# First block of a chunked linear-attention kernel: scores in three quarters, one mask a tile, outputs by early, then by late keys

## Chip, cores and metric

One core of one Trainium2 chip. The metric is the device time of one execution in microseconds; of several runs the median is taken. A lower time is better.

## What is computed

The reference is a gated linear attention over 4 batches x 8 heads, 768 tokens, head width 48, and behind it two pairs of dense layers over all 3072 tokens:

```python
for t in range(S):
    state = alpha[:, :, t, :, None] * state + einsum('bhd,bhe->bhde', k[:, :, t], v[:, :, t])
    y[:, :, t] = einsum('bhd,bhde->bhe', q[:, :, t], state)
x = y.transpose(0, 2, 1, 3).reshape(B * S, H * D)         # 3072 x 384
h = x @ w_in;  g = h * clip(h + 3, 0, 6) / 6;  x = g @ w_out      # 384 -> 2048 -> 384
h = x @ w_in2; g = max(h, 0) ** 2;             out = g @ w_out2
```

## The kernel before

**Attention by tiles.** The recurrence is computed in chunks of tokens. `k` and `q` are scaled with running products of the decays, so that inside a chunk `y = (mask of q k^T) v` and between chunks a 48 x 48 state is carried on. There are 18 tiles. Tiles 0 to 3 (`t < BATCH`) are the first block: one tile a batch, with the first 128 tokens of all 8 heads. Tiles 4 to 17 are scored in pieces of 64 tokens, between the steps of the first dense layer. The heads lie in pairs: the even one on rows 0 to 47, the odd one on rows 64 to 111 (`half_rows`). In `k`, `v` and the decays the 128 tokens stand in reversed order, in `q` in natural order. So keys 0 to 63 of a tile are its late keys and 64 to 127 its early ones.

**One tile of the first block.**
- VectorE: `make_decays` (L692 to L713), two scans along the tokens with a reciprocal between them; `scale_keys` for tiles 0 and 3 (L719) and `scale_queries` (L726). GpSimd scales the keys of tiles 1 and 2 (L512).
- TensorE: `score` (L895), 16 matmuls in fp32: per pair of heads, half of the keys (64 of 128 output partitions) and head of the pair one matmul of 48 rows x 64 keys with 128 queries. Even and odd heads go to two PSUM banks. `turn_keys` (L965): four transposes of the keys into a third bank.
- VectorE: `mask` (L744), two multiplications of 128 x 512, one a bank, with the 128 x 128 triangle `causal`, from PSUM to SBUF.
- ScalarE: `copy_keys` (L559) out of PSUM, `check_from_end` and `check_to_token` (L547, L553), which square all decays and add them up for a check of their range, each with a read of its accumulator.
- TensorE: `attend_first` (L973), for each of three groups of output rows four matmuls of all 128 keys x 64 rows with 128 queries; tiles 0 to 2 put all three groups in the bank of their even scores, tile 3 uses three banks. `add_up_first` (L1000): eight matmuls for the tile's state.
- ScalarE: `x_high` or, for tile 3, `last_x_high` (L565) rounds the output to fp32r; `first_state` (L585) copies the state, twice 48 x 192. VectorE: `x_low` and `last_x_low` (L771) take the rest.

**The dense layers.** 96 steps a layer (6 blocks of 512 tokens x 16 groups of 128 hidden columns). A step has `hidden(g)` (L1025, nine fp32r matmuls of 512 columns into `h_ps[g % 2]`) and `project(g - 2)` (L1055, nine more). Between them ScalarE makes `gate(g)` (L592) from PSUM, VectorE the product `activate(g)` (L783), ScalarE its high part `high(g)` (L601), GpSimd its low part `low(g)` (L520). `hidden(g)` waits for `activate(g - 2)`. The weights come in eight groups by DMA; each is split by ScalarE (`split_w`, L619) into a high part and by GpSimd (groups 0 and 1) or VectorE into a low part. `hidden(0)` to `hidden(3)` need group 0, `project(0)` group 1.

**What sets the order.** Each engine runs a list written out by hand and waits only on semaphores: TensorE at L1087 to L1125, VectorE at L832 to L850, ScalarE at L631 to L650, GpSimd at L530 to L535, and SP's queue of transfers at L448 to L480. TensorE's list for the first block is

```python
warm_up(0); score(0); turn_keys(0); warm_up(1); attend_first(0); add_up_first(0)
score(1); turn_keys(1); warm_up(2); attend_first(1); add_up_first(1)
score(2); turn_keys(2); wait_ge(masked, 2); warm_up(3); add_up_first(2)
score(3); turn_keys(3); attend_first(2); attend_first(3); add_up_first(3); hidden(0) ...
```

`warm_up(i)` (L891) issues `WARM_UP[i]` matmuls of 128 x 128 x 128 whose results nobody reads. SP loads tile 6 and later ones into slots of earlier tiles; it waits for both checks and the outputs of the tile that had the slot (`load_tile`, L394).

## Time and profile before

| what | value |
|---|---|
| time, median of 3 runs | 858.87 us (858.85 to 859.05) |
| the profiled execution | 859.79 us, span 858.0 us |
| granted TensorE clock | 1.0 of full speed in all 40 slices |
| TensorE (matmuls) busy | 849.1 us, 99% of the span |
| VectorE busy | 331.7 us, 39% |
| ScalarE busy | 327.7 us, 38% |
| GpSimd busy | 312.0 us, 36% |
| first block, 7.56 to 26.65 us | TensorE 16.89 busy, VectorE 17.28, ScalarE 10.87, GpSimd 8.04 |

The span runs from the first to the last instruction of the profiled execution; the execution's own time has the start and the end around it. "Busy" is the time in which an engine has an instruction in work. A timeline row gives the start, the length from the first start to the last end, the engine, the line of the kernel, the operation, output <- inputs, how many instructions the row stands for, and in brackets the idle time before it with what ended it. The ends of matmuls are modelled, and matmuls overlap: the next start can lie ahead of the end of the one before. An fp32 matmul of the program is two instructions.

### The profile page before, as it was taken

The page shows a single profiled execution, that of the slowest core. Times are in us where ns is not written, and L with a number is a line of the kernel's source. Part 1 is how long each engine was busy: PE and PEld are TensorE (multiplying, and loading weights), DVE is VectorE, ACT ScalarE, POOL GpSimd, SP SyncE. Part 2 cuts the span into 40 slices and gives each one's busy share as a digit, 9 for nine tenths or more (in the row PEclk, how much of TensorE's full clock was granted, in tenths as well). Part 3 has the DMA queues.
Part 4 walks back from the last instruction along what each step waited for, and adds up shares of the span by engine and source line. Part 5 has one row for each costly group of instructions (what it writes and reads, how often), then busy time and mean ns, then how long its engine had stood idle before and what let it go on. Part 6 is the DMA issues. An engine that isn't in the chain of part 4 may idle for free.

```text
span 858.0 us, 15319 instructions
## 1 busy us (share of the span) xinstructions
PE 849.1 (99%) x6312; PEld 703.3 (82%) x6312; DVE 331.7 (39%) x468; ACT 327.7 (38%) x586; POOL 312.0 (36%) x246
## 2 busy tenths in 40 slices
PE   7999999999999999999999999999999999999998
PEld 7888888888888888888888888888888888888886
DVE  8887545564455555421333311212211211211111
ACT  4664433343433334333445433333333333323332
POOL 2655443343443443433333333333333333333332
PEclk9999999999999999999999999999999999999999
DMA  9743233332223332200323001000000000100101
GB/s 347 299 109 94 42 91 90 90 77 74 70 78 103 80 86 75 61 16 5 111 74 111 0 1 38 1 0 25 14 1 7 30 1 0 37 1 1 37 0 39
DMA packets 67496, 51.84 MB, mean 60 GB/s; under 512 B 50785, under 2 KB 57185, under 8 KB 67425
## 3 DMA queue, kind: packets, MB, share of 16 engines
...
## 4 chain that ended last, share of the span: by engine, by line
PE 97%; DMA 1%; SPq 0%; ACT 0%; issue 0%; ACTq 0%
PE h_ps L1051 46%; PE o_ps L1064 46%; PE att_all L944 1%; DMA w_in_raw<-w_in 1%; PE att_all L928 1%; PE att_all L995 1%; PE att_all L1019 1%; SPq L400 0%; PE h_ps L981 0%; ACT k_tok L562 0%; PE att_all L906 0%; SPq L406 0%; PE att_all L981 0%; SPq L402 0%; ACT squares L550 0%
## 5 line engine op out<-in xcount | busy, mean ns | idle before, releaser
L522 POOL TENSOR_TENSOR g_parts<-h_act,g_parts 128x512 fp32r<-128x512 f32 x192 | 256.5, 1336 | 523.9 <-ACT g_parts L604 523.8
L1064 PE MATMUL o_ps<-g_parts,w_out_hi 128*128 128x512 f32 x1152 | 327.1, 389 | 0.0
L1051 PE MATMUL h_ps<-x_parts,w_in_hi 128*128 128x512 f32 x1152 | 295.3, 392 | 0.0
L1064 PEld LDWEIGHTS o_ps<-g_parts,w_out_hi 128*128 128x128 f32 x1152 | 216.2, 188 | 45.0
L1051 PEld LDWEIGHTS h_ps<-x_parts,w_in_hi 128*128 128x128 f32 x1152 | 214.4, 188 | 45.3
L604 ACT ACTIVATE g_parts<-h_act 128x512 fp32r<-128x512 f32 x192 | 121.4, 632 | 272.9 <-PE o_ps L1064 241.0
L790 DVE SCALAR_TENSOR_TENSOR h_act<-h_ps,h_gate 128x512 f32<-128x512 f32 x96 | 66.3, 691 | 290.5 <-ACT h_gate L599 290.5
L1064 PE MATMUL o_ps<-g_parts,w_out_lo 128*128 128x512 f32 x576 | 165.6, 389 | 0.0
L1051 PE MATMUL h_ps<-x_parts,w_in_lo 128*128 128x512 f32 x576 | 161.9, 389 | 0.0
L1051 PEld LDWEIGHTS h_ps<-x_parts,w_in_lo 128*128 128x128 f32 x576 | 108.1, 188 | 22.6
L1064 PEld LDWEIGHTS o_ps<-g_parts,w_out_lo 128*128 128x128 f32 x576 | 108.1, 188 | 22.4
L787 DVE SCALAR_TENSOR_TENSOR h_act<-h_gate,h_ps 128x512 f32<-128x512 f32 x96 | 65.3, 680 | 141.0 <-ACT h_gate L596 141.0
L599 ACT ACTIVATE h_gate<-h_ps 128x512 f32<-128x512 f32 x96 | 57.4, 598 | 110.8 <-PE h_ps L1051 110.8
L596 ACT ACTIVATE h_gate<-h_ps 128x512 f32<-128x512 f32 x96 | 57.2, 596 | 109.2 <-PE h_ps L1051 109.1
L708 DVE TENSOR_TENSOR_SCAN inputs<-inputs,seeds 112x520 f32<-112x520 f32 x18 | 37.0, 2056 | 0.6
L768 DVE TENSOR_TENSOR tails<-att_all,tails 112x128 fp32r<-112x128 f32 x20 | 5.8, 292 | 57.7 <-ACT x_parts L583 57.7
L700 DVE TENSOR_TENSOR_SCAN inputs<-inputs,seeds 112x520 f32<-112x520 f32 x18 | 22.4, 1242 | 1.9
L512 POOL TENSOR_TENSOR inputs<-inputs 112x512 f32<-112x512 f32 x17 | 20.6, 1213 | 0.0
L517 POOL TENSOR_TENSOR inputs<-inputs 112x512 f32<-112x512 f32 x17 | 20.4, 1197 | 0.0
L810 DVE TENSOR_TENSOR x_parts<-x_mid,x_parts 128x1536 fp32r<-128x1536 f32 x6 | 10.6, 1759 | 18.3 <-ACT x_parts L625 18.3
L741 DVE STREAM_TRANSPOSE x_mid<-inputs 128x512 f32<-128x512 f32 x16 | 17.5, 1092 | 0.0
L944 PEld LDWEIGHTS att_all<-inputs,state 48*48 48x48 f32 x576 | 11.3, 120 | 6.6 <-issue 6.3
...
## 6 DMA issues: line engine op xcount, KB each, us to landing
...
```

Source lines behind the costliest of these rows:

```text
L512: nc.gpsimd.tensor_tensor(by_chunk(t, keys(t)), by_chunk(t, keys(t)), from_end(t)[:, :, 0:chunk(t)], ALU.mult).then_inc(k_scaled, 1)
L517: nc.gpsimd.tensor_tensor(by_chunk(t, queries(t)), by_chunk(t, queries(t)), to_token(t)[:, :, 0:chunk(t)], ALU.mult).then_inc(q_scaled, 1)
L522: nc.gpsimd.tensor_tensor(g_parts[:, g % 2, 1, :], h_act[:, g % 2, :], g_parts[:, g % 2, 0, :].bitcast(F32), ALU.subtract).then_inc(g_lo, 1)
L596: nc.scalar.activation(h_gate[:, g % 2, :], h_ps[g % 2][:, :], ACT.Relu, bias=0.5, scale=1.0 / 6.0).then_inc(gate_made, 1)
L599: nc.scalar.activation(h_gate[:, g % 2, :], h_ps[g % 2][:, :], ACT.Relu).then_inc(gate_made, 1)
L604: nc.scalar.activation(g_parts[:, g % 2, 0, :], h_act[:, g % 2, :], ACT.Copy).then_inc(g_hi, 1)
L700: nc.vector.tensor_tensor_scan(scanned(t, ATT_W), scanned(t, KQ_W), other_seeds(t), 0.0, ALU.mult, ALU.max).then_inc(from_end_made, 1)
L708: nc.vector.tensor_tensor_scan(loaded[:, ::-1], loaded[:, ::-1], other_seeds(t), 0.0, ALU.mult, ALU.max).then_inc(to_token_made, 1)
L787: nc.vector.scalar_tensor_tensor(h_act[:, g % 2, :], h_gate[:, g % 2, :], 1.0, h_ps[g % 2][:, :], ALU.min, ALU.mult).then_inc(act_made, 1)
L790: nc.vector.scalar_tensor_tensor(h_act[:, g % 2, :], h_ps[g % 2][:, :], 0.0, h_gate[:, g % 2, :], ALU.max, ALU.mult).then_inc(act_made, 1)
L1051: last = nc.tensor.matmul(h_ps[g % 2][:, :], w[:, m, cols], x_parts[:, n % 2, part, m, :], start=m == 0 and i == 0, stop=m == KT - 1 and i ...
L1064: return nc.tensor.matmul(o_ps[m][:, :], w[:, f, m * P:(m + 1) * P], g_parts[:, g % 2, part, :], start=f == 0 and w is w_out_hi and part = ...
```

## The change

- **Scores in three quarters.** `score` leaves out the quarter of late keys by early queries, which the mask makes zero. The other three are written as three kinds, one after the other: late keys by late queries, early keys by early queries, both to columns 0 to 255 of the tile's two banks (on partitions 0 to 63 and 64 to 127), then early keys by late queries to columns 256 to 511. Within a kind it goes over the four pairs and their two heads: 24 matmuls of 64 columns, with one `scored` at the end of either bank.
- **One mask.** VectorE multiplies both diagonal quarters of both banks in one operation of 128 x 512 with the 64 x 64 triangles `causal_part`. ScalarE's new `copy_cross` copies the third quarter (64 x 512) to SBUF, after the mask. `causal` and its two GpSimd operations are gone.
- **Outputs in two passes.** `attend_first` first does the 12 matmuls of the early keys (64 rows, all 128 queries), then waits for them (`early_attended`) and adds the 12 of the late keys (64 rows, 64 late queries) to the same sums. Tile 3, with its banks of its own, waits group by group. It also waits for `cross_copied`.
- **Order.** TensorE: `warm_up(3)` and its wait for `masked` go; `turn_keys(2)`, `turn_keys(3)`, `score(3)`, `add_up_first(2)` follow each other. ScalarE: the four `copy_cross`; `split_w(0)` behind `copy_cross(1)`, `split_w(1)` behind the last high part, `check_to_token(1)` behind `first_state(3)`, and the checks of tiles 2 and 3 one step of the first layer later.
- **Banks.** All of PSUM is one tensor, and the first block's scores, keys, sums and outputs are given to other banks (`FIRST_BANKS`, `FIRST_Y_BANK`, `LAST_Y_BANKS`). Outputs: tile 0's in the bank of its odd scores, tile 2's in the one of its even scores.

```diff
--- before.py
+++ after.py
...
+BANK = 512
+H_BANK, O_BANK, ATT_BANK = 0, 2, 5
...
+FIRST_BANKS = ((ATT_BANK, ATT_BANK + 1, ATT_BANK + 2), (O_BANK + 1, O_BANK + 2, O_BANK), (H_BANK, H_BANK + 1, ATT_BANK + 2),
+               (O_BANK + 2, ATT_BANK, O_BANK))
+FIRST_Y_BANK = (ATT_BANK + 1, O_BANK + 1, H_BANK)
+LAST_Y_BANKS = (H_BANK + 1, O_BANK + 2, ATT_BANK)
 SCORES_W = PAIRS * PART
...
-WARM_UP = (14, 8, 3, 2)
+WARM_UP = (14, 8, 3)
...
-            return pairs(banks(t)[2][half_rows(half), 0:PAIRS * HD])
...
+        def bank(n):
+            return banks[:, n * BANK:(n + 1) * BANK]
+        def first_bank(t, i):
+            return bank(FIRST_BANKS[t][i])
+        def first_scores(t, rows, first):
+            even, odd = FIRST_BANKS[t][0:2]
+            part = banks[rows, even * BANK + first:even * BANK + first + SCORES_W]
+            return bass.AP(part.tensor, part.offset, [part.ap[0], [(odd - even) * BANK, 2], [PART, PAIRS], [1, PART]])
         def first_y(t, m):
-            bank = (att_ps[1], o_ps[1], att_ps[0])[m] if t == BATCH - 1 else banks(t)[0]
-            return bank[:, m * TILE:(m + 1) * TILE]
+            return bank(LAST_Y_BANKS[m] if t == BATCH - 1 else FIRST_Y_BANK[t])[:, m * TILE:(m + 1) * TILE]
...
         def by_part(ap):
             return ap.rearrange("p m (a q) -> p m a q", a=2)
+        LATE, EARLY = slice(0, PART), slice(PART, TILE)
...
+        cross_copied = sem("cross_copied")
+        early_attended = sem("early_attended")
...
             nc.gpsimd.memset(ident[:], 0.0).then_inc(init_pool, 1)
-            nc.gpsimd.memset(causal[:], 1.0).then_inc(init_pool, 1)
-            pool.wait_ge(init_pool, 2)
+            pool.wait_ge(init_pool, 1)
             nc.gpsimd.affine_select(out=ident[:], in_=ident[:], compare_op=ALU.not_equal, fill=1.0, base=0,
                                     pattern=[[-1, P]], channel_multiplier=1).then_inc(init_pool, 1)
-            nc.gpsimd.affine_select(out=causal[:], in_=causal[:], compare_op=ALU.is_ge, fill=0.0, base=1 - TILE,
-                                    pattern=[[1, TILE]], channel_multiplier=1).then_inc(init_pool, 1)
-            pool.wait_ge(init_pool, 4)
+            pool.wait_ge(init_pool, 2)
             nc.gpsimd.memset(state[:, :, :, :], 0.0).then_inc(state_cleared, 1)
             nc.gpsimd.memset(causal_part[:], 1.0).then_inc(part_ready, 1)
             pool.wait_ge(part_ready, 1)
...
                 past(act, u_made, t)
-                nc.scalar.activation(k_tok[:, :, :], banks(t)[2][:, 0:PAIRS * ROWS].rearrange("p (a b) -> p a b", a=PAIRS),
+                nc.scalar.activation(k_tok[:, :, :], first_bank(t, 2)[:, 0:PAIRS * ROWS].rearrange("p (a b) -> p a b", a=PAIRS),
                                      ACT.Copy).then_inc(k_back_copied, 1)
+            def copy_cross(t):
+                act.wait_ge(masked, 2 * (t + 1))
+                nc.scalar.activation(masked_of(t)[EARLY, :, :, PART:TILE], first_scores(t, EARLY, SCORES_W), ACT.Copy).then_inc(cross_copied, 1)
...
             copy_keys(0)
             check_from_end(0)
             check_to_token(0)
+            copy_cross(0)
             x_high(0)
             first_state(0)
-            split_w(0)
             copy_keys(1)
             check_from_end(1)
-            check_to_token(1)
+            copy_cross(1)
+            split_w(0)
             x_high(1)
             first_state(1)
             copy_keys(2)
-            split_w(1)
+            copy_cross(2)
+            copy_cross(3)
             copy_keys(3)
             x_high(2)
             for m in range(KT):
                 last_x_high(m)
+            split_w(1)
             first_state(2)
             first_state(3)
-            check_from_end(2)
+            check_to_token(1)
             for g in range(2 * STEPS + LAG):
                 n, f = divmod(g, FT)
                 if g < 2 * STEPS:
                     gate(g)
                     if g == 0:
+                        check_from_end(2)
+                    if g == 1:
                         check_to_token(2)
-                    if g == 1:
+                    if g == 2:
                         check_from_end(3)
-                    if g == 2:
+                    if g == 3:
                         check_to_token(3)
...
             def mask(t):
-                for half in range(2):
-                    dve.wait_ge(scored, 2 * t + half + 1)
-                    past(dve, y_made, t - 1)
-                    nc.vector.tensor_tensor(masked_of(t)[:, half, :, :], pairs(banks(t)[half][:, :]),
-                                            causal[:, :].unsqueeze(1).broadcast_to([P, PAIRS, TILE]), ALU.mult).then_inc(masked, 1)
+                dve.wait_ge(part_ready, 3)
+                dve.wait_ge(scored, 2 * (t + 1))
+                past(dve, y_made, t - 1)
+                nc.vector.tensor_tensor(masked_of(t)[:, :, :, 0:PART], first_scores(t, slice(0, P), 0),
+                                        causal_part[:, :].unsqueeze(1).unsqueeze(1).broadcast_to([P, 2, PAIRS, PART]),
+                                        ALU.mult).then_inc(masked, 2)
             def mask_later(t):
-                if t == BATCH:
-                    dve.wait_ge(part_ready, 3)
                 dve.wait_ge(scored, pieces_of(t))
                 dve.wait_ge(y_made, t)
...
-            dve.wait_ge(init_pool, 4)
...
             def warm_up(i):
-                for _ in range(WARM_UP[i]):
-                    nc.tensor.matmul((att_ps[1] if i == 3 else h_ps[0])[:, 0:P], ident[:, :], ident[:, :], start=True, stop=True)
+                for n in range(WARM_UP[i]):
+                    place = att_ps[n // 2][:, 256 + n % 2 * P:256 + (n % 2 + 1) * P] if i == 0 and n < 4 else h_ps[0][:, 0:P]
+                    nc.tensor.matmul(place, ident[:, :], ident[:, :], start=True, stop=True)
...
             def score(t):
-                bank_even, bank_odd, _ = banks(t)
                 pe.wait_ge(k_scaled, t + 1)
                 pe.wait_ge(q_scaled, t + 1)
                 if t == BATCH - 1:
                     pe.wait_ge(masked, 2 * (t - 1))
-                for j in range(PAIRS):
-                    for part in range(2):
-                        cols = slice(HALF * part, HALF * (part + 1))
-                        for half, bank in enumerate((bank_even, bank_odd)):
+                    pe.wait_ge(cross_copied, t - 1)
+                for kind, (keys_of, queries_of, first) in enumerate(((LATE, slice(PART, TILE), 0), (EARLY, slice(0, PART), 0),
+                                                                     (EARLY, slice(PART, TILE), SCORES_W))):
+                    for j in range(PAIRS):
+                        for half in range(2):
                             rows = half_rows(half)
-                            last = nc.tensor.matmul(bank[cols, j * TILE:(j + 1) * TILE], keys(t)[rows, j, cols],
-                                                    queries(t)[rows, j, :], start=True, stop=True)
-                            if j == PAIRS - 1 and part == 1:
+                            last = nc.tensor.matmul(first_bank(t, half)[keys_of, first + j * PART:first + (j + 1) * PART],
+                                                    keys(t)[rows, j, keys_of], queries(t)[rows, j, queries_of], start=True, stop=True)
+                            if kind == 2 and j == PAIRS - 1:
                                 last.then_inc(scored, 1)
...
             def turn_keys(t):
-                bank_k = banks(t)[2]
+                pe.wait_ge(k_scaled, t + 1)
+                bank_k = first_bank(t, 2)
                 if t >= 2:
                     pe.wait_ge(state_made, 2 * (t - 1))
                 for j in range(PAIRS):
...
             def attend_first(t):
                 wait_values(pe, t)
                 pe.wait_ge(masked, 2 * (t + 1))
+                pe.wait_ge(cross_copied, t + 1)
                 for m in range(KT):
-                    if t == BATCH - 1 and m == KT - 1:
-                        pe.wait_ge(x_lo, 1)
                     for kind, j in enumerate((m, TAIL)):
                         for half in range(2):
                             last = nc.tensor.matmul(first_y(t, m)[HALF * half:HALF * (half + 1), :],
-                                                    first_values(t)[:, kind, m, half, :], masked_of(t)[:, side_of(j, half), j, :],
-                                                    start=kind == 0, stop=kind == 1)
+                                                    first_values(t)[EARLY, kind, m, half, :], masked_of(t)[EARLY, side_of(j, half), j, :],
+                                                    start=kind == 0 and (m == 0 or t == BATCH - 1), stop=True, skip_group_check=True)
+                    last.then_inc(early_attended, 1)
+                for m in range(KT):
+                    pe.wait_ge(early_attended, KT * t + (m + 1 if t == BATCH - 1 else KT))
+                    for kind, j in enumerate((m, TAIL)):
+                        for half in range(2):
+                            last = nc.tensor.matmul(first_y(t, m)[HALF * half:HALF * (half + 1), PART:TILE],
+                                                    first_values(t)[LATE, kind, m, half, :], masked_of(t)[LATE, side_of(j, half), j, 0:PART],
+                                                    start=False, stop=True, skip_group_check=True)
                     if t == BATCH - 1 and m < KT - 1:
                         last.then_inc(last_y_made, 1)
                 last.then_inc(y_made, 1)
...
-            pe.wait_ge(init_pool, 4)
+            pe.wait_ge(init_pool, 2)
             pe.wait_ge(init_vec, 1)
             warm_up(0)
             score(0)
...
             add_up_first(1)
             score(2)
             turn_keys(2)
-            pe.wait_ge(masked, 2)
-            warm_up(3)
+            turn_keys(3)
+            score(3)
             add_up_first(2)
-            score(3)
-            turn_keys(3)
             attend_first(2)
             attend_first(3)
             add_up_first(3)
...
```

## Rows read from the trace of the kernel before

**Rows 1.** Page, parts span and 1: busy time and share of each engine.

```profile
span 858.0 us, 15319 instructions
...
PE 849.1 (99%) x6312; PEld 703.3 (82%) x6312; DVE 331.7 (39%) x468; ACT 327.7 (38%) x586; POOL 312.0 (36%) x246
```

**Rows 2.** TensorE's waits from 22 us on: total us, times, longest.

```profile
PE att_all L928 <- PE att_all L995: 0.2, 1, 0.2
```

**Rows 3.** Timeline of TensorE, 0 to 46 us: start, length, instructions, idle before.

```profile
7.56 1.10 PE L906 MATMUL att_all<-x_mid 48*64 48x128 f32 x32 [0.66 <-DVE x_mid L726]
8.59 0.60 PE L970 MATMUL att_all<-ident,x_mid 112*128 112x112 f32 x4
...
11.58 1.53 PE L981 MATMUL att_all<-masked_t,first_v 128*64 128x128 f32 x24 [0.58 <-DVE masked_t L748]
12.91 0.56 PE L1009 MATMUL att_all<-first_v,k_tok 128*48 128x48 f32 x16
13.40 1.10 PE L906 MATMUL o_ps<-x_mid 48*64 48x128 f32 x32
...
16.39 1.53 PE L981 MATMUL o_ps<-h_gate,first_v 128*64 128x128 f32 x24 [0.67 <-DVE h_gate L748]
...
20.50 0.62 PE L893 MATMUL att_all<-ident 128*128 128x128 f32 x4
...
26.20 0.53 PE L1009 MATMUL o_ps<-first_v,k_tok 128*48 128x48 f32 x16
26.65 1.65 PE L1051 MATMUL h_ps<-x_parts,w_in_hi 128*128 128x512 f32 x6
...
30.86 1.52 PE L1051 MATMUL h_ps<-x_parts,w_in_hi 128*128 128x512 f32 x6
...
44.31 0.63 PE L995 MATMUL att_all<-masked_t,inputs 64*48 64x64 f32 x32
45.13 0.70 PE L928 MATMUL att_all<-inputs 48*64 48x64 f32 x32 [0.19 <-PE att_all L995]
45.62 0.43 PE L944 MATMUL att_all<-inputs,state 48*48 48x64 f32 x16
```

**Rows 4.** The same timeline inside the scores of tile 3.

```profile
22.12 0.27 PE L906 MATMUL att_all<-x_mid 48*64 48x128 f32 x1
...
22.14 0.27 PE L906 MATMUL o_ps<-x_mid 48*64 48x128 f32 x1
22.23 0.27 PE L906 MATMUL att_all<-x_mid 48*64 48x128 f32 x1
```

**Rows 5.** Timeline of VectorE: masks, and products of the first layer.

```profile
10.17 1.26 DVE L748 TENSOR_TENSOR masked_t<-att_all,causal 128x512 f32<-128x512 f32 x2
...
14.98 1.26 DVE L748 TENSOR_TENSOR h_gate<-o_ps,causal 128x512 f32<-128x512 f32 x2
...
29.66 0.69 DVE L787 SCALAR_TENSOR_TENSOR h_act<-h_gate,h_ps 128x512 f32<-128x512 f32 x1 [0.61 <-ACT h_gate L596]
...
33.89 0.67 DVE L787 SCALAR_TENSOR_TENSOR h_act<-h_gate,h_ps 128x512 f32<-128x512 f32 x1
...
41.88 0.68 DVE L756 TENSOR_TENSOR masked_t<-att_all,causal_part 128x512 f32<-128x512 f32 x1
```

**Rows 6.** Timeline of ScalarE: key copy, check, gate, weight split.

```profile
9.30 0.54 ACT L562 ACTIVATE k_tok<-att_all 128x448 f32<-128x448 f32 x1 [6.99 <-PE att_all L970]
...
11.09 0.19 ACT L556 ACTIVATION_READ_ACCUMULATOR squares<-x_mid 112x1 f32 x1
...
29.02 0.60 ACT L596 ACTIVATE h_gate<-h_ps 128x512 f32<-128x512 f32 x1 [0.33 <-PE h_ps L1051]
...
35.14 1.47 ACT L621 ACTIVATE w_in_hi<-w_in_raw 128x1536 fp32r<-128x1536 f32 x1
```

**Rows 7.** Timeline of GpSimd: the low part of a weight group.

```profile
24.41 3.48 POOL L527 TENSOR_TENSOR w_out_lo<-w_out_raw,w_out_hi 128x1536 fp32r<-128x1536 f32 x1
```

**Rows 8.** Line L708 by form, VectorE's second scan: lengths min/median/max in ns.

```profile
L708 DVE TENSOR_TENSOR_SCAN inputs<-inputs,seeds x18: 1241/2239/2242, 30.5 to 357.4; 112x520 f32<-112x520 f32 x18
```

22 lines of the change are left out of this document (9 added, 13 removed).

## Prediction

> **What bounds the kernel now.** The page comes first. TensorE is busy for 99% of the span [rows 1]. Its waits from 22 us to the end hold one entry, 0.2 us [rows 2]. So everything from the first product of the first layer, `hidden(0)` at 26.65 us, to the end is TensorE's own work, which the change leaves alone. An edit of the first block can move the time in two ways: it shifts the start of `hidden(0)`, or it makes one of the first steps behind it wait.
>
> Next, TensorE's timeline up to 26.65 us [rows 3]. It is nearly full: the idle bits in front of the first scores and the outputs of tiles 0 and 1 are 0.66, 0.58 and 0.67 us, and warm-ups, such as the one of 0.62 at 20.50 which the change drops, fill time that nothing else wanted. Their end-to-start order shows the pace: scores, key turn, warm-up, wait for the mask, outputs, sums, next scores. VectorE runs in a closed line beside it [rows 5]: the first mask starts at 10.17 although its scores ended at 8.66, the second at 14.98 although its scores ended at 14.50. Up to there VectorE sets the pace. From the scores of tile 3 on TensorE has no gap at all [rows 2]. So both engines are near the limit in this stretch, and the question is which one the change loads.
>
> **Unit prices of TensorE.** The matmuls of the scores start four at a time, every 0.11 us [rows 4]: the four quarters of the array (two key-row halves by two output halves) run side by side, and each quarter takes one instruction of 128 columns in 0.107 us. An fp32 matmul is two instructions (16 matmuls are x32). 64 columns take half: 32 instructions of `score_later`, eight a quarter, go from 45.13 to the next start at 45.62 [rows 3], 0.43 us at 0.053 each plus a little. The outputs use two quarters' worth at a time (all 128 rows, two column halves): 24 instructions, 12 a half, 12 x 0.107 = 1.28 us, and 11.58 to 12.91 shows 1.33.
>
> **Scores.** Before: 32 instructions over four quarters, 8 x 0.107 = 0.86; start to next start 1.03 [rows 3]. After: 24 matmuls, 48 instructions of 64 columns. But the kind is the outer loop, and within a kind all go to one output half, so only two quarters work: 24 x 0.053 = 1.28, less one pair that overlaps where late keys give way to early ones: 1.23. So each score costs 0.37 to 0.38 more, though it computes a quarter less. Start to next is 1.41, start to ready 1.48 instead of 1.10.
>
> **Outputs, the largest term.** Before 1.33. After, the early keys' pass has 64 rows but still 128 columns and two column halves: 1.28, its last result at +1.53 (its row's length). Then TensorE waits for its own semaphore `early_attended`. The one such wait in the trace, `attended` before `score_later`, left it idle 0.19 us after the drained end (44.31 + 0.63 to 45.13) [rows 2, 3]. Late keys' pass: 24 instructions of 64 columns on two quarters, 12 x 0.053 = 0.64. Sum: 1.53 + 0.19 + 0.64 = 2.36. Behind it the sums use another division of the array than these 64-row pieces. Such changes cost: from scores to key turn it is 1.03 for 0.86 of work, some 0.15 [rows 3]. The Trainium skill says the same ("TensorEngine Tiling (Array Packing)", Key Properties: a change of tiling mode drains the engine); without it the sum would be 0.15 x 4 = 0.6 smaller. So start to next is 2.51, +1.18 for each of tiles 0, 1 and 2, all queued in front of the tile's sums and the next tile's scores. Tile 3 has a bank for each output and waits only for the same `m`, so no drain: 1.28 + 0.64 + 0.15 = 2.07 against 1.31, +0.75.
>
> **VectorE.** Two multiplications a tile, 1.26 us, become one of as many elements as `mask_later` has, 0.68 at 41.88 [rows 5]: 0.6 less a tile, four times. That pays only where VectorE sets the pace.
>
> **ScalarE.** `copy_cross`: 512 elements out of PSUM as in `gate`, 0.60 [rows 6], and it waits for the whole mask. So the path from scores to outputs is not shorter: 0.68 + 0.04 + 0.60 + 0.06 against 1.26 + 0.15. It is also queued behind the key copy and one or both checks. Before, from a key copy to the end of both checks it took 9.30 to 11.28, 1.89 to the next start [rows 6].
>
> **The line through the first block**, each time from the ones before:
> - scores(0) start at 7.56 as now (VectorE's queries). Next start 8.97, keys turned 9.57.
> - ScalarE: key copy 9.62, checks, `copy_cross(0)` 11.51 to 12.11. Outputs(0) 12.17 (11.58 now). The mask was ready at 10.85, so the ScalarE queue decides here.
> - Sums(0) 14.68, scores(1) 15.17 (13.40 now), ready 16.65. VectorE could have masked at 14.40 and stands idle for 2.3 us: TensorE is the pace now. Mask(1) 16.70 to 17.38.
> - Keys(1) turned 17.18; ScalarE: copy 17.22 and one check, 1.06 for both (0.44 for the copy, its length of 0.54 less the overlap, and less than half of what is left of the 1.89, since the wait between two checks falls away), `copy_cross(1)` 18.28 to 18.88. Outputs(1) 18.94 (16.39 now).
> - Sums(1) 21.45, scores(2) 21.94 (sums take 0.49 as 12.91 to 13.40), key turns(2, 3) 23.35, scores(3) 24.30 (two turns of 0.60 less overlap and a change of division),  sums(2) 25.71, outputs(2) 26.20. Beside this VectorE, from mask(1) at 16.70, is ready for mask(2) after the 4.81 that lie between the masks now [rows 5], less 0.6 for the halved mask and plus 0.6 for its own keys of tile 3: 21.5, before scores(2) are ready at 23.42. Mask(3) starts at 25.8, and its copy ends at 27.2, before outputs(3) wants it.
> - Outputs(3) 28.56, sums(3) 30.63, `hidden(0)` 31.08 with the 0.45 now seen from 26.20 to 26.65.
>
> Shift of `hidden(0)`: 31.08 - 26.65 = **+4.4 us**. The warm-up of 0.62 that is dropped and the lost idle bits are in this already. A check by adding up: 4 x 0.38 + 3 x 1.18 + 0.75 = 5.8, plus 0.6 and 0.8 that ScalarE's queue adds in front of outputs(0) and (1), less some 2.8 of warm-up and idle time that are eaten.
>
> **The first steps behind it.** ScalarE now has `split_w(1)` (1.47 long, 1.38 to the next, as the split at 35.14 [rows 6]) between the last high part and `first_state(2)`. Before, `gate(0)` started at 29.02, 2.37 after `hidden(0)`, of which 0.33 was idle: the queue was ready at +2.04. In the line above the last high part falls 0.1 earlier against `hidden(0)` than now, so the queue is ready at 2.04 + 1.38 - 0.1 = +3.3. `gate(0)` ends at +3.9, VectorE's product at +4.6, TensorE may go at +4.75, and `hidden(2)` was due at +4.21 (30.86 [rows 3]): 0.5 lost. VectorE then has the decays of tile 4 before the next product (29.66 to 33.89, 4.23 apart [rows 5]), so `hidden(3)` loses another 0.1. GpSimd's low part of that weight group (3.48 [rows 7]) starts at +1.5 and ends at +5.0, before `project(0)`, which comes after a third hidden product at +6.7. The two checks moved a step later, and the checks that SP's loads of tiles 6 and 7 wait for, cost nothing: tile 6's load needs tile 0's checks and outputs alone, and tile 7's stands in SP's queue behind `store_turned(4)`, which needs work of the first layer's fourth step, when tile 1's late check (34 us) is long done. GpSimd's shorter start gives TensorE its first warm-up 0.4 us earlier, which ends in more waiting for VectorE at 7.56: nothing.
>
> **Sum.** 4.4 + 0.6 = +5.0 us. The profiled execution took 859.79 us for a span of 858.0; the median of the runs is 858.87, 0.92 lower. By the profile: span 863.0, execution 864.8. By the median: 858.87 + 5.0 = **863.9 us**.
>
> **Unknown prices.** The wait for its own pass: nothing, if it drains beside other work, to twice the 0.44 (0.25 of drain, 0.19 idle): -1.3 to +1.3 over three tiles; I take the row, the same kind of wait. Change of division: 0 to 0.19: -0.6 to +0.2. Steps behind `hidden(0)`: 0 to 1.4, since VectorE's second scan may run beside GpSimd, where most of its kind took 2.24 instead of 1.24 [rows 8]. One output half with two row halves never runs alone in this trace: between four quarters' pace (0.64 a score, below now) and none side by side (2.5); I take two, since the four starts of a group include such pairs.
>
> **Rivals.**
> - *The late pass does not wait* (chance 0.14): drain and change of division hidden. Then outputs cost 1.33 + 0.64, `hidden(0)` comes near 29.5 and the time is 862.3. For it: starts overlap the ends before them everywhere. Against it: the one self-wait in the trace did idle.
> - *Not slower* (0.12): the parts that use different rows run side by side, late keys beside early ones, in scores and outputs. This decides once a tile's outputs cost no more than 1.33 and a score 0.82. Then VectorE stays the pace and its 0.6 a tile counts: the same line gives `hidden(0)` at 24.6 for both, 26.95 if only the outputs gain. With 0.6 behind it: 857.4 to 859.8. The Trainium skill gives the principle ("TensorE: Matmul & The Clock Gate", Part 3: matmuls on different row groups run at the same time). Against it: the late pass adds to the same sums and has a wait ahead of it, and the starts go in program order with the kind outermost. Only tile 3 has its own banks, and there I let the passes overlap.
> - *ScalarE and VectorE late in the first layer* (0.08): the scan beside GpSimd adds 0.8 to the product that `hidden(3)` wants, and the queue of copies adds as much again: 865.7.
>
> My forecast has 0.66. Its own range is 862.9 to 865.0. The range that holds 8 in 10 reaches to the first rival's lower half and to the third's time: 861.0 to 865.7. A measurement of this kernel can tell 0.2%, 1.7 us. Faster by more: 0.04 (the lower end of the second rival). Within: 0.08. Slower: 0.88.
>
> **What would show it.** Right: outputs of tiles 0 to 2 in two groups with about 0.2 us of idle time released by TensorE itself; each score 1.4 to the next start; VectorE idle more than 1.5 us before mask(1), released by TensorE; `hidden(0)` near 31.1; a wait of about half a microsecond of `hidden(2)` for VectorE. Wrong: late matmuls that start beside early ones in tiles 0 to 2, scores in under 1 us, or `hidden(0)` before 27.

## The result and the profile after

The changed kernel took **875.66 us** (median of 6, 867.90 to 876.97), the kernel before 858.94 in the same comparison: a ratio of 1.016, interval 1.013 to 1.019. It is slower, as forecast, but by 16.7 us in the median where 5.0 was forecast, and outside the range of 861.0 to 865.7.

The six times fall into two groups, and the granted TensorE clock goes with them:

```
us      867.90  868.09  874.75  876.57  876.86  876.97
clock   1.000   1.000   0.986   0.982   0.982   0.982
```

Executions of the kernel before, seven of them listed with the first experiments, all had 1.000 (the 24 listed with the later ones had 0.999 or 1.000). The granted clock is the one that TensorE was given, averaged over the execution, as a share of full speed (2.4 GHz). The profiled execution is the one of 867.90 us. Its page [rows 1]:

```profile
span 866.2 us, 15633 instructions
...
PE 854.8 (99%) x6468; PEld 708.0 (82%) x6468; DVE 331.0 (38%) x464; ACT 330.3 (38%) x590; POOL 312.2 (36%) x244
```

TensorE's waits from 10 us on, total, times, longest, without the one entry of 0.2 us that [rows 2] had and that is still there:

```profile
PE banks L1010 <- ACT h_gate L585: 1.3, 1, 1.3
PE banks L1010 <- ACT masked_t L585: 1.0, 1, 1.0
PE banks L1010 <- issue: 1.0, 1, 1.0
PE banks L934 <- issue: 0.8, 1, 0.8
PE banks L1088 <- DVE h_act L813: 0.8, 2, 0.4
```

Two entries name "issue": TensorE waited for nothing that the profile shows. The forecast had neither. They are called the unnamed gaps from here on.

TensorE's timeline, the counterpart of [rows 3] (L934 scores, L999 key turn, L1010 early pass, L1018 late pass, L1046 sums, L1088 `hidden`):

```profile
7.56 1.44 PE L934 MATMUL banks<-x_mid 48*64 48x64 f32 x48 [0.61 <-DVE x_mid L753]
8.94 0.60 PE L999 MATMUL banks<-ident,x_mid 112*128 112x112 f32 x4
...
12.38 1.53 PE L1010 MATMUL banks<-masked_t,first_v 64*64 64x128 f32 x24 [1.04 <-ACT masked_t L585]
13.96 0.92 PE L1018 MATMUL banks<-masked_t,first_v 64*64 64x64 f32 x24
14.81 0.56 PE L1046 MATMUL banks<-first_v,k_tok 128*48 128x48 f32 x16
15.30 1.44 PE L934 MATMUL banks<-x_mid 48*64 48x64 f32 x48
...
19.23 1.78 PE L1010 MATMUL banks<-h_gate,first_v 64*64 64x128 f32 x24 [1.27 <-ACT h_gate L585]
...
22.42 1.44 PE L934 MATMUL banks<-x_mid 48*64 48x64 f32 x48
...
24.70 0.44 PE L934 MATMUL banks<-x_mid 48*64 48x64 f32 x7
25.91 1.21 PE L934 MATMUL banks<-x_mid 48*64 48x64 f32 x41 [0.76 <-issue]
...
32.16 0.32 PE L1010 MATMUL banks<-h_gate,first_v 64*64 64x128 f32 x1 [0.97 <-issue]
...
33.52 1.66 PE L1088 MATMUL banks<-x_parts,w_in_hi 128*128 128x512 f32 x6
...
38.21 1.67 PE L1088 MATMUL banks<-x_parts,w_in_hi 128*128 128x512 f32 x6 [0.32 <-DVE h_act L813]
...
43.06 1.66 PE L1088 MATMUL banks<-x_parts,w_in_hi 128*128 128x512 f32 x6 [0.43 <-DVE h_act L813]
```

`hidden(0)` starts at 33.52 instead of 26.65: +6.9, where +4.4 was forecast. `hidden(2)` and `hidden(3)` are idle for 0.32 and 0.43 us before they start. Up to the scores of tile 2 the forecast line holds within half a microsecond: 8.94 (8.97), 12.38 (12.17), 15.30 (15.17), 19.23 (18.94), 22.42 (21.94). It breaks inside the scores of tile 3: seven instructions from 24.70, then nothing until 25.91. A second gap lies in front of 32.16, inside the outputs of tile 3. The early pass of tile 1 at 19.23 is also 0.25 longer than that of tile 0 (1.78 for 1.53).

VectorE's mask of tile 1 [rows 5]; the idle time before it was forecast at 2.3 us and is 1.85, released by TensorE:

```profile
16.92 0.69 DVE L775 TENSOR_TENSOR h_gate<-banks,causal_part 128x512 f32<-128x512 f32 x1 [1.85 <-PE banks L934]
```

ScalarE [rows 6]: `copy_cross(0)`, `split_w(1)`, `gate(0)`:

```profile
11.64 0.59 ACT L585 ACTIVATE masked_t<-banks 64x512 f32<-64x512 f32 x1
...
33.32 1.48 ACT L643 ACTIVATE w_out_hi<-w_out_raw 128x1536 fp32r<-128x1536 f32 x1
...
36.83 0.60 ACT L618 ACTIVATE h_gate<-banks 128x512 f32<-128x512 f32 x1
```

`gate(0)` starts 3.31 us after `hidden(0)`, as forecast (+3.3). So the profiled execution has the forecast mechanism, plus two unnamed gaps, and four of six executions have something else besides.

### The profile page after: what moved, and what is told of

It reads as the page before. It is cut to its first block, busy times and chain, and to the rows that moved or that the text cites. A ratio compares the mean times of both kernels' runs of the same rounds, so it can differ in the third digit from the quotient of the medians.

```text
span 866.2 us, 15633 instructions
## 1 busy us (share of the span) xinstructions
PE 854.8 (99%) x6468; PEld 708.0 (82%) x6468; DVE 331.0 (38%) x464; ACT 330.3 (38%) x590; POOL 312.2 (36%) x244
## 4 chain that ended last, share of the span: by engine, by line
PE 97%; DVE 1%; ACT 1%; issue 1%; DMA 0%; ACTq 0%
PE banks L1088 45%; PE banks L1101 45%; PE banks L972 1%; PE banks L956 1%; PE banks L1032 1%; PE banks L1056 1%; PE banks L1010 1%; PE banks L934 1%; PE banks L1018 0%; DMA x_mid<-att_in 0%; PE banks L999 0%; DVE inputs L735 0%; DVE inputs L746 0%; PE banks L1046 0%; ACT squares L573 0%
## 5 line engine op out<-in xcount | busy, mean ns | idle before, releaser
L1101 PE MATMUL banks<-g_parts,w_out_hi 128*128 128x512 f32 x1152 | 327.1, 389 | 0.0
L1088 PE MATMUL banks<-x_parts,w_in_hi 128*128 128x512 f32 x1152 | 295.7, 392 | 0.8 <-DVE h_act L813 0.8
L1101 PEld LDWEIGHTS banks<-g_parts,w_out_hi 128*128 128x128 f32 x1152 | 216.3, 188 | 44.8
L1088 PEld LDWEIGHTS banks<-x_parts,w_in_hi 128*128 128x128 f32 x1152 | 214.4, 188 | 46.7 <-DVE h_act L813 1.6
L816 DVE SCALAR_TENSOR_TENSOR h_act<-banks,h_gate 128x512 f32<-128x512 f32 x96 | 66.3, 691 | 290.5 <-ACT h_gate L621 290.5
L1101 PE MATMUL banks<-g_parts,w_out_lo 128*128 128x512 f32 x576 | 165.7, 389 | 0.0
L1088 PE MATMUL banks<-x_parts,w_in_lo 128*128 128x512 f32 x576 | 162.0, 390 | 0.0
L1088 PEld LDWEIGHTS banks<-x_parts,w_in_lo 128*128 128x128 f32 x576 | 108.2, 188 | 22.7
L1101 PEld LDWEIGHTS banks<-g_parts,w_out_lo 128*128 128x128 f32 x576 | 108.2, 188 | 22.5
L621 ACT ACTIVATE h_gate<-banks 128x512 f32<-128x512 f32 x96 | 57.5, 599 | 110.8 <-PE banks L1088 110.8
L618 ACT ACTIVATE h_gate<-banks 128x512 f32<-128x512 f32 x96 | 57.3, 597 | 107.9 <-PE banks L1088 107.9
L972 PEld LDWEIGHTS banks<-inputs,state 48*48 48x48 f32 x576 | 11.3, 120 | 6.6 <-issue 6.3
```

The source lines that it names most:

```text
L618: nc.scalar.activation(h_gate[:, g % 2, :], h_ps[g % 2][:, :], ACT.Relu, bias=0.5, scale=1.0 / 6.0).then_inc(gate_made, 1)
L621: nc.scalar.activation(h_gate[:, g % 2, :], h_ps[g % 2][:, :], ACT.Relu).then_inc(gate_made, 1)
L816: nc.vector.scalar_tensor_tensor(h_act[:, g % 2, :], h_ps[g % 2][:, :], 0.0, h_gate[:, g % 2, :], ALU.max, ALU.mult).then_inc(act_made, 1)
L1088: last = nc.tensor.matmul(h_ps[g % 2][:, :], w[:, m, cols], x_parts[:, n % 2, part, m, :], start=m == 0 and i == 0, stop=m == KT - 1 and i ...
L1101: return nc.tensor.matmul(o_ps[m][:, :], w[:, f, m * P:(m + 1) * P], g_parts[:, g % 2, part, :], start=f == 0 and w is w_out_hi and part = ...
```

## Experiments

Twelve experiments ran. Those named a_ are the changed kernel again or edits of it, those named b_ edits of the kernel before. Three things were to be settled: the unnamed gaps, the clock, and how the forecast's own terms share the rest.

### a_again: the changed kernel once more, to see a trace at the low clock

> The changed kernel once more, unchanged. Its times so far lie in two groups, 867.9 to 868.1 us at a granted clock of 1.000 and 874.8 to 877.0 at 0.982 to 0.986. Theory: the 8.8 us between the groups is one stretch of TensorE at 1.2 GHz that begins in the first 40 us; expected again both groups, and, if the profiled execution is one of the slow ones, a stretch in its trace in which a product of 512 columns takes about 0.43 us instead of 0.23. Rival: the runs differ in something else (transfers, the end of the kernel) and the mean clock only goes with it; then the low clock is spread or lies late.

Four executions: 876.68, 876.51, 873.15 and 868.54 us at clocks of 0.982, 0.982, 0.988 and 0.995. The profiled one was the first. Its time in stretches (the columns after the busy times are granted clock, DMA share, GB/s):

```profile
12.00:14.00 2.00, 1.31 (x24) 1.31 (x24) 1.82 (x5) 0.55 (x1) 0.00 (x0) 1.00 0.97 382
14.00:16.00 2.00, 1.94 (x38) 1.61 (x36) 1.07 (x1) 0.32 (x1) 0.84 (x1) 0.63 1.05 406
16.00:40.00 24.00, 23.22 (x322) 21.14 (x322) 8.01 (x13) 7.95 (x16) 3.77 (x2) 0.50 0.90 354
...
44.00:46.00 2.00, 2.00 (x8) 1.58 (x7) 0.37 (x1) 1.34 (x4) 2.00 (x1) 0.69 0.01 4
46.00:60.00 14.00, 14.00 (x92) 11.36 (x91) 13.06 (x16) 10.24 (x20) 8.60 (x5) 1.00 0.01 2
```

TensorE's rows at both ends of the stretch:

```profile
12.69 1.53 PE L1010 MATMUL banks<-masked_t,first_v 64*64 64x128 f32 x24 [1.03 <-ACT masked_t L585]
14.28 1.36 PE L1018 MATMUL banks<-masked_t,first_v 64*64 64x64 f32 x24
...
42.43 2.93 PE L1088 MATMUL banks<-x_parts,w_in_hi 128*128 128x512 f32 x6
...
45.89 1.53 PE L1088 MATMUL banks<-x_parts,w_in_hi 128*128 128x512 f32 x6
```

The early pass of tile 0 at 12.69 has its full-clock length (1.53), the late pass at 14.28 takes 1.36 for 0.92. From 14.6 the granted clock is 0.50 (1.2 GHz) until 45.2. All the small matmuls of the first block run at it, 322 of them from 16 to 40 us with TensorE busy for 23.22 of 24 us, and in this execution none brings the clock back. It comes back behind the first six products of 128 rows, 128 columns of weights and 512 columns of data (2.93 for them at 42.43, 1.53 at 45.89). `hidden(0)` starts at 42.43 instead of 33.52, and the span is 8.8 longer. The rival (a difference elsewhere in the kernel) falls: the shift of `hidden(0)` is 8.9 and that of the end 8.8. Two things do differ besides. The first warm-up takes 6.21 us where the other profiled execution has 5.21, and the first scores start 0.32 later. And the unnamed gaps (1.7 us idle) and the two waits of `hidden(2)` and `hidden(3)` (0.75 us) are gone in this execution, so that the slow stretch costs more than 8.8 by itself. That the gaps are gone because TensorE consumes its code more slowly is a likely reason, not tested by itself.

### a_held: no weight transfers beside the first block

```diff
             load_values(4)
+            sp.wait_ge(y_made, BATCH)
             load_w(2)
             load_w(3)
```

> The changed kernel with SP's queue held before load_w(2) until tile 3's outputs are made, so that no weight transfers run beside the first block from about 20 us on. Theory (instruction fetch): the two idle stretches that TensorE's rows put down to nothing (0.8 us inside the scores of tile 3, 1.0 us inside its outputs) are instruction blocks of 16 KB that come late through busy DMA engines; with the engines free both vanish and hidden(0) starts near 31.4 us instead of 33.5. The later steps keep their time unless a weight group comes late, so 866 us in the fast group. Rival (a wait for another engine or for sums that the profile doesn't name): both idle stretches stay as they are, hidden(0) at 33.5.

In the profiled execution (865.39 us, clock 1.0), scores of tile 3 and `hidden(0)`:

```profile
24.68 1.44 PE L935 MATMUL banks<-x_mid 48*64 48x64 f32 x48
...
31.14 1.66 PE L1089 MATMUL banks<-x_parts,w_in_hi 128*128 128x512 f32 x6
```

Both gaps are gone; the 48 instructions of the scores are in one piece, and `hidden(0)` starts at **31.14**. The forecast had 31.08. The span is 2.5 us shorter than the changed kernel's. Instruction blocks have a queue of their own in the trace. One of the changed kernel's, from 23.0 to 23.5 us (packets, MB, share of 16 engines' time):

```profile
q8 instruction: 1, 0.02, 12.9%
```

In quarters of a microsecond, such packets show from 16.0, 23.25 and 29.5 us in the changed kernel, with the DMA engines full (a share of 1.03 from 16 to 32 us); in a_held from 16.0, 20.75, 24.75 and 29.5, with a share of 0.24 from 20 to 25 us. The gaps end at 25.91 and 32.16, 2.7 us behind the packets' start. Between the two gaps lie 127 matmuls with a weight load each, 254 instructions. The Trainium skill describes this ("Runtime: NRT & Kernel Launch", Instruction fetch mechanics: an engine's code is refilled in blocks of 16 KiB, 256 instructions); the trace agrees with the size (0.02 MB a packet) and nearly with the spacing. The same section calls the cost mostly hidden; here `hidden(0)` came 2.4 us later for it. The long early pass of tile 1 (1.78), whose slack lies some 124 matmuls ahead of the first gap, looks like a third and smaller one. It stays in a_held, where the DMA engines are still full up to 20 us. The other three executions still fell to 0.989, 0.988 and 0.982 (871.72 to 876.80 us), so the hold does nothing for the clock.

### a_four: diagonal quarters of the scores interleaved

```diff
-                for kind, (keys_of, queries_of, first) in enumerate(...):
-                    for j in range(PAIRS):
-                        for half in range(2):
+                for j in range(PAIRS):
+                    for keys_of, queries_of in ((LATE, slice(PART, TILE)), (EARLY, slice(0, PART))):
+                        for half in range(2):
+                            piece(j, half, keys_of, queries_of, 0)
+                for j in range(PAIRS):
+                    for half in range(2):
+                        last = piece(j, half, EARLY, slice(PART, TILE), SCORES_W)
```

> The changed kernel with the late and the early diagonal quarter of the scores interleaved pair by pair, so that four quarters of the array work for two thirds of the matmuls. Theory (a kind has only two quarters of the array): a score takes 1.05 us to the next start instead of 1.38, because 16 matmuls of 64 columns on four quarters take 0.43 and the other 8 on two take 0.43; hidden(0) about 0.9 to 1.2 us earlier if no instruction block is later for it, else the gain is lost in longer idle stretches. Rival (the number of instructions sets the pace, 48 at some 29 ns): the score stays at 1.38 to 1.44 us.

Scores of tile 0 and what follows:

```profile
7.62 1.16 PE L931 MATMUL banks<-x_mid 48*64 48x64 f32 x48 [0.67 <-DVE x_mid L753]
8.72 0.60 PE L1004 MATMUL banks<-ident,x_mid 112*128 112x112 f32 x4
```

1.10 to the next start instead of 1.38, with as many instructions. So the forecast's price was right: a kind by itself has only two of the array's quarters, and two instructions side by side take 0.053 us. Of four times 0.28, `hidden(0)` gained 0.83 (32.69), and the gap in the scores of tile 3 grew from 0.76 to 0.96. Times: 867.35, 867.38, 867.60 at 0.998 and 871.95 at 0.988. In the profiled execution the clock fell at 32.9, beside the first products of the dense layer, and was back at 36.3. Three of the four executions lost so little; whether the denser scores are the reason was not tested.

### b_more: more instructions in the warm-ups of the kernel before

```diff
-                for _ in range(WARM_UP[i]):
-                    nc.tensor.matmul(...[:, 0:P], ident[:, :], ident[:, :], ...)
+                pieces = 4 if i else 1
+                for _ in range(WARM_UP[i] * pieces):
+                    nc.tensor.matmul(...[:, 0:P // pieces], ident[:, :], ident[:, 0:P // pieces], ...)
```

> The kernel before with warm_up(1) to (3) in pieces of 32 columns, 52 matmuls in place of 13 of 128 columns: the same columns, 78 trace matmuls (156 instructions) more. Theory (instruction fetch): the block boundary falls into the scores or outputs of tile 3 and TensorE idles there for 0.3 to 1.5 us with nothing named as the cause, so the time is 859.2 to 860.4 us, and some executions may fall to a lower clock. Rival (no fetch limit): no unnamed idle stretch, 858.9 us plus at most 0.5 for the overhead of small matmuls.

869.31 us median, and it tests nothing of instruction fetch. Each of the added matmuls has a load of 128 columns of weights. At full clock 24 of them took 2.78 us (0.116 each), about what one of 128 columns takes (16 in 1.96, 0.122 each). `warm_up(1)`, with 64 for 16, took 9.04 us, and the clock fell in it:

```profile
9.60 9.04 PE L894 MATMUL h_ps<-ident 128*128 128x32 f32 x64
18.57 2.83 PE L982 MATMUL att_all<-masked_t,first_v 128*64 128x128 f32 x24
```

TensorE was slower by more than the added code could make up, and no unnamed gap appeared. The expectation had priced the columns and not the weight loads. The run shows something else, though: the granted clock is at 0.50 from 14.8 to 21.5 us, and TensorE had stood idle nowhere between 8.12 us and that fall. It came back while the outputs and sums of tile 0 ran, on all 128 rows.

### a_fill: longer warm-ups in front of the outputs of tiles 0 and 1

```diff
-WARM_UP = (14, 8, 3)
+WARM_UP = (14, 12, 8)
```

> The changed kernel with warm_up(1) of 12 matmuls instead of 8 and warm_up(2) of 8 instead of 3, which fills 0.85 of the 1.04 us and 1.07 of the 1.27 us that TensorE stands idle before the outputs of tiles 0 and 1. Theory (those idle bits, beside matmuls that use half of the array's rows, let the clock fall to 1.2 GHz): granted clock 1.000 in all executions or nearly all, 867 to 869 us each, no group at 875. The nine matmuls more put the late instruction blocks a little earlier in the code, so the two unnamed idle stretches stay at 0.8 to 1.5 us. Rival (the short and narrow matmuls alone are too little activity, whatever lies between them): most executions still at 0.98 to 0.99 and 872 to 877 us.

**866.02 us**, four executions from 865.83 to 866.32, all at a clock of 1.000; a little under the expected 867, since the late blocks cost less too. Nine matmuls whose results nobody reads take 9.6 us off the median. The early pass of tile 1, with 0.16 us of idle time before it instead of 1.27, and `hidden(0)`:

```profile
19.33 1.53 PE L1010 MATMUL banks<-h_gate,first_v 64*64 64x128 f32 x24 [0.16 <-ACT h_gate L585]
...
31.61 1.64 PE L1088 MATMUL banks<-x_parts,w_in_hi 128*128 128x512 f32 x6
```

Waits, of which only the second unnamed gap is left, and half as long:

```profile
PE banks L1010 <- issue: 0.4, 1, 0.4
```

`hidden(0)` at 31.61 is nearly a_held's, with full DMA engines. A likely reason: the filler runs in time that was idle, so TensorE reaches the end of a code block earlier, and the next one is asked for earlier. The traces bear it out. The instruction packets show from 12.0, 19.25 and 26.75 us instead of 16.0, 23.25 and 29.5. And the gap that is left lies 18 matmul instructions earlier in the code than the second one before, which is just what nine more matmuls of two instructions each move a block's end by. So the gaps go with a place in the code and not with a certain wait. As to the clock, a_fill ran on another chip than the changed kernel in a_again. But on a third chip a_split (below), with these warm-ups and other edits besides, had 0.999 to 1.000 in all four executions, and a_fill_one, without the longer second warm-up, fell to 0.988 in two of four.

### a_fill_one: only the first warm-up longer

```diff
-WARM_UP = (14, 8, 3)
+WARM_UP = (14, 12, 3)
```

> The changed kernel with warm_up(1) alone lengthened, 12 matmuls for 8; the 1.27 us of idle time before the outputs of tile 1 stay. Theory: either idle bit is enough to let the clock fall, so some executions still end up at 0.985 to 0.99 (the fall comes at about 21 us instead of 14.5) and 870 to 875 us. Rival: the first bit, near the start of the full clock, is what counts; then all stay at 1.000 and 866 to 868 us.

865.70 and 865.78 us at 1.000 and 0.999, 872.94 and 873.27 at 0.988. So the clock still falls in some executions with the second idle bit (1.27 us) alone; no slow one of this kernel was profiled, so the place of the fall isn't shown. In the profiled one (865.70) four more matmuls did as much against the unnamed gaps as holding the transfers back: packets from 12.25, 19.25 and 26.75 us, no "issue" among the waits, the early pass of tile 1 in 1.53 and

```profile
31.16 1.67 PE L1088 MATMUL banks<-x_parts,w_in_hi 128*128 128x512 f32 x6
```

with the DMA engines as full as before (shares of 1.00 to 1.07 from 16 to 36 us).

### b_cold and b_two_cold: idle time with and without the narrower matmuls

```diff
-WARM_UP = (14, 8, 3, 2)
+WARM_UP = (14, 0, 3, 2)
```

> The kernel before without warm_up(1), so that TensorE stands idle for some 2.5 us before the outputs of tile 0. Theory (an idle stretch in the first block makes the clock fall, and the first block's own matmuls don't bring it back): the clock falls to 1.2 GHz there and stays there until the products of the dense layer, as in the slow executions of the changed kernel; mean clock about 0.98 to 0.99 and 862 to 868 us. Rival (only the changed kernel's 64-row pieces keep the clock down): the clock is back within the first block, and the time is 859 to 861 us.

The theory as I had put it fell: 858.97 us (10 executions, 858.73 to 860.20), clock 0.998 to 1.000, although TensorE is idle for 2.39 us before the outputs of tile 0. Four of the ten had 0.998 and 859.62 to 860.20 us, the others at most 858.98, so the clock may have fallen for a short stretch in those; none of them was profiled. Idle time alone does not keep it down. The same edit on b_two (below), where nothing but the outputs differs from b_cold:

> The kernel before with outputs in two passes (b_two) and without warm_up(1). b_two alone never left the full clock, and the kernel before without warm_up(1) hardly did. Theory: it takes both, idle time of more than a microsecond and matmuls on half of the rows behind it; then the clock falls in most executions and stays at 1.2 GHz until the dense layer, mean clock 0.98 to 0.99, 866 to 872 us. Rival (the scores on two quarters keep it down, not the outputs): clock 0.998 to 1.000 and 861.5 to 864 us.

870.54 us median (864.83 at 0.996, the other three 870.41 to 870.75 at 0.988):

```profile
12.00:16.00 4.00, 3.94 (x50) 3.42 (x47) 3.02 (x5) 0.00 (x0) 0.72 (x1) 0.50 1.04 403
16.00:30.00 14.00, 13.93 (x168) 12.12 (x170) 7.03 (x11) 6.64 (x14) 3.89 (x2) 0.50 1.03 404
30.00:34.00 4.00, 4.00 (x70) 3.44 (x70) 1.37 (x3) 1.47 (x2) 3.00 (x1) 0.70 1.05 407
```

The clock is down from 12.0, just behind the start of the outputs of tile 0 (11.72), and comes back at 32.4, at the end of the scores of tile 3, which here still use all four quarters. The same scores of tiles 1 and 2 had not brought it back. b_two itself, with its idle bits of 0.59 and 0.27 us, had 1.000 in all six executions. So in these kernels it takes both: the idle time of 2.4 us, and behind it the outputs in two passes on half of the rows. Two things limit this. b_two and b_cold ran on one chip and b_two_cold on another, so that a difference between chips isn't excluded here. And it is no rule: in b_more the clock fell with no idle time and all rows in use. And the two passes differ from the one in more than their rows, they also take 1.1 us longer, so which of it counts isn't separated.

### b_two: the kernel before with outputs in two passes

```diff
-    first_values(t)[:, kind, m, half, :], masked_of(t)[:, side_of(j, half), j, :], ...
+    first_values(t)[PART:TILE, kind, m, half, :], masked_of(t)[PART:TILE, side_of(j, half), j, :], ...
+    last.then_inc(early_attended, 1)
+for m in range(KT):
+    pe.wait_ge(early_attended, ...)
+    ... first_y(t, m)[..., PART:TILE], first_values(t)[0:PART, ...], masked_of(t)[0:PART, ..., PART:TILE]
```

> The kernel before with one part of the change alone: outputs in two passes of 64 keys, the second over the 64 late queries after a wait for the first. Scores, masks and ScalarE's queue as before. Theory: each of tiles 0 to 2 takes 2.45 instead of 1.33 us for its outputs, tile 3 2.0 instead of 1.3; VectorE's line still sets the masks of tiles 0 and 1, so about half of 4.1 us is eaten by the warm-ups' and waits' room: hidden(0) at 29.0 to 30.0 instead of 26.65, 861.4 to 862.6 us at clock 1.000. Rival (the scores and the ScalarE copies cost most of the 4.5 us): hidden(0) before 28 and under 860.5 us. If the clock falls in some executions here too, it is the 64-row outputs that bring it about, not the copies' waits.

862.10 us (862.02 to 862.62), ratio 1.0036 (1.0024 to 1.0049). Outputs of tile 0 in two passes, sums, and `hidden(0)`:

```profile
11.67 1.53 PE L982 MATMUL att_all<-masked_t,first_v 64*64 64x128 f32 x24 [0.59 <-DVE masked_t L749]
...
14.10 0.56 PE L1018 MATMUL att_all<-first_v,k_tok 128*48 128x48 f32 x16
...
29.22 1.65 PE L1060 MATMUL h_ps<-x_parts,w_in_hi 128*128 128x512 f32 x6
```

2.43 to the sums (11.67 to 14.10) where the forecast had 2.51, and `hidden(0)` 2.6 later. This one part costs 3.1 us (862.10 against 859.03); the whole change was forecast at 5.0.

### a_between: sums between the two passes

```diff
                     last.then_inc(early_attended, 1)
+                if between:
+                    add_up_first(t)
                 for m in range(KT):
```

with the hold of a_held and the warm-ups of a_fill.

> The changed kernel with the held weight transfers, the longer warm-ups of a_fill, and the sums of tiles 0 to 2 issued between the early and the late pass of the outputs, so that they stand in for the drain. Theory (the pass of late keys waits 0.19 us beyond the drained end of the early pass, some 0.4 us of TensorE in all, for each of three tiles): outputs and sums of a tile together take 2.45 to 2.5 us instead of 2.92 (12.38 to 15.30), hidden(0) at 30.0 to 30.4 instead of 31.14 us, clock 1.000, 864.0 to 864.8 us. Rival (the self-wait costs nothing beyond the pipeline's end, or two changes of the array's division eat the gain): hidden(0) at 30.9 or later and 865 us.

864.63 us (864.60 to 864.93), clock 1.000. Tile 0, early pass, sums, late pass, next scores:

```profile
12.68 1.53 PE L1011 MATMUL banks<-masked_t,first_v 64*64 64x128 f32 x24
14.13 0.56 PE L1049 MATMUL banks<-first_v,k_tok 128*48 128x48 f32 x16
14.63 0.85 PE L1021 MATMUL banks<-masked_t,first_v 64*64 64x64 f32 x21
...
15.37 1.40 PE L935 MATMUL banks<-x_mid 48*64 48x64 f32 x47
```

12.68 to 15.37 is 2.69 for outputs and sums, where the changed kernel needs 2.92 (12.38 to 15.30). `hidden(0)` comes at 30.38 instead of 31.14. The time around the self-wait (TensorE's wait for its own early pass) is real and can be filled, but the saving is 0.23 in tile 0 and not 0.4. The expectation's 2.45 to 2.5 had left out the two changes of the array's division, which is a likely reason and was not tested; its start for `hidden(0)` was met, in part because tile 1's early pass took 1.53 here and 1.78 in a_held.

### a_split: split_w(1) moved in front of x_high(2)

```diff
             copy_keys(3)
+            split_w(1)
             x_high(2)
             for m in range(KT):
                 last_x_high(m)
-            split_w(1)
```

> a_between with ScalarE's split_w(1) moved from behind the last high part to in front of x_high(2), where ScalarE stood idle. Theory: the two waits of hidden(2) and hidden(3) for VectorE (0.30 and 0.49 us, with the drained pipeline about 1.1 us together) come from the ScalarE queue in front of gate(0) alone; both go, hidden(0) stays at 30.4, and the time falls from 864.6 to 863.5 us. Rival (VectorE itself is late with the decays of tile 4): the second wait stays, 864.1 us or more.

863.70 us (863.43 to 863.80) after 864.63 in a_between. TensorE's waits, apart from the first, are now three, of 0.4, 0.2 and 0.2 us, and none of them is one of `hidden(2)` or `hidden(3)` for VectorE. The place of the split in ScalarE's queue cost 0.9 us, nearly all of it behind `hidden(0)` (30.25 for 30.38).

### a_all: all repairs together

```diff
             check_from_end(0)
+            copy_cross(0)
             check_to_token(0)
-            copy_cross(0)
             ...
-WARM_UP = (14, 8, 3)
+WARM_UP = (14, 10, 5)
```

and the edits of a_held, a_four, a_between and a_split.

> All repairs of the changed kernel together: held weight transfers, sums between the passes, diagonal quarters of the scores interleaved, split_w(1) in front of x_high(2), copy_cross(0) and (1) in front of the last check, warm-ups of 10 and 5. By the line of times: outputs(0) 11.65, scores(1) 14.3, outputs(1) 17.25, scores(2) 19.9, scores(3) 21.9, outputs(3) 25.45, hidden(0) 27.9 us against 26.65 in the kernel before, no wait behind it. Theory: 860.2 us (859.6 to 861.0), clock 1.000, still slower than before, since TensorE's two passes cost 0.64 a tile more than VectorE's relief is worth. Rival (VectorE was what held the first block, and the relief counts once the queues are in order): under 858.5 us.

862.13 us median; four executions lie from 861.38 to 862.79 at 1.000, one at 862.69 (0.999) and one at 867.33 (0.994). Outputs of tiles 0 and 1, and `hidden(0)`:

```profile
11.65 1.53 PE L1016 MATMUL banks<-masked_t,first_v 64*64 64x128 f32 x24
...
17.33 1.53 PE L1016 MATMUL banks<-h_gate,first_v 64*64 64x128 f32 x24 [0.21 <-ACT h_gate L586]
...
28.08 1.66 PE L1096 MATMUL banks<-x_parts,w_in_hi 128*128 128x512 f32 x6
```

The expected line had 11.65, 17.25 and 27.9, but the profiled execution took 861.38 us where 860.2 was expected. So the line is right, and the mapping to the time a microsecond too good: I had taken the start of `hidden(0)` in the profiled execution before, 26.65, for that of the median, and that execution lay 0.9 us above the median. With all queues in order the change is still 2.4 us slower in its best execution and 3.1 in the median. No version that beats the kernel before was found.

## Why the prediction failed

**Where the 16.7 us are.** The profiled execution of 867.90 us lies 9.0 above the median before. Against the profiled execution before, `hidden(0)` is 6.9 later and 1.3 is lost behind it, 8.2 together; that execution was itself 0.9 above its median. Of the 6.9, 4.5 are the forecast line (31.14 in a_held against 26.65), and 2.4 the late instruction blocks. The median lies another 7.8 above 867.90, since most executions have a stretch at 1.2 GHz.

| term | forecast | measured | by |
|---|---|---|---|
| line of scores, outputs and copies up to `hidden(0)` | +4.4 | +4.5 | a_held |
| late instruction blocks | - | +2.4 | a_held |
| first steps of the dense layer | +0.6 | +1.3 | after; 0.9 of it a_split |
| profiled execution before, above its median | - | +0.9 | before |
| clock at 1.2 GHz in most executions | - | +7.8 in the median | a_again, a_fill |

The rows are rounded. The last one is the net of the fall: 8.8 in the span of a_again, in which the gaps and the waits of the first steps are gone. Against a_held's profiled execution, which has no such gaps, a_again is 11.3 longer.

**Step by step.**
- *What bounds the kernel*: right that TensorE and not VectorE is the pace, and that the line of TensorE's work up to `hidden(0)` is what counts. Wrong in what it took as given: TensorE's prices of [rows 3] hold only at the clock of that trace and with the code at hand. This is the step that failed: a fall of the clock and late code were terms put at nothing, without a reason. The runs showed in their place a granted clock of 0.50 from 14.6 to 45.2 us in a_again, 8.8 us of its span, and 2.4 us of late code. Warm-ups were read as filling "time that nothing else wanted"; in this kernel they also keep up the clock. a_fill shows it at a cost of nine matmuls: 866.02 for 875.66 us.
- *Scores*: +0.35 to the next start (1.38 against 1.03), forecast +0.38. Shown by a_four.
- *Outputs*: +1.10 (2.43 against 1.33), forecast +1.18. The self-wait: the late pass starts 1.58 behind the early one (12.38 to 13.96), so it idles by 0.05 and not by 0.19 past the modelled end. Tile 3 overlapped its passes as forecast (1.97 to its sums in a_held, forecast 2.07).
- *ScalarE*: `copy_cross(0)` at 11.64 (11.51), outputs(0) 12.38 (12.17): ScalarE's copy reaches TensorE 0.15 us after its end, not 0.06. The idle bits that it left, 1.04 and 1.27 us, were in the forecast's line (outputs(0) 0.6 later, the warm-up's length unchanged), but priced at nothing beyond themselves.
- *VectorE*: the masks were halved as forecast (0.67 for 1.26), but the query scaling behind mask(0) took 1.47 for 0.87, so the idle time in front of mask(1) is 1.85 and not 2.3. TensorE was the pace there, so it cost nothing.
- *From the line to the time*: the forecast took +5.0 to the median, 858.87, and dropped the 864.8 that it had by the profile. But its line gives times of the trace, and 26.65 is from an execution 0.9 above the median. So the forecast would have been short even at full clock and without gaps: a_fill_one's better executions took 865.7. In [rows 3] that trace also has waits for ScalarE's key copies that the text does not count, 0.61 and 0.34 us in front of the sums of tiles 1 and 2; b_cold's trace has only the second, 0.31.
- *The first steps behind it*: `gate(0)` as forecast at +3.3. The two waits cost 0.6 and 0.75 us, counting that the first products behind a wait take longer to follow each other (1.51 to the next group for 1.37), forecast 0.5 and 0.1: VectorE's scan took 1.87 beside GpSimd's split, the bound that the forecast had named and not taken.
- *Rivals*: that the late pass waits for nothing, or that passes run side by side, are both out by b_two. None of the rivals had the clock or the code, and the widest bound stopped at +6.8. A price for slow matmuls could have been read in the trace before: the 28 of its first warm-up average 0.355 us, the longest has 0.579, and later ones take 0.275. The granted clock reads 1.00 there too, so the trace did not give the cause.

**What stays open.** How much idle time and how narrow a matmul it takes was not measured, and b_more shows a fall without idle time. Why the clock falls in some executions of one kernel and not in others is open; in the two profiled ones of the changed kernel the first warm-up differed by 1.0 us. Why a_four falls less is open too. The experiments were spread over three chips, and no edited kernel was timed on two of them; only the kernel before was, which kept 0.999 to 1.000 on each. No run had more code and no more work at a full clock, since b_more did not do that; the fetch rests on a_held, the packets' times, the spacing of the gaps and the 18 matmul instructions by which a_fill moved the second.
